# Attention in front of two layers of experts: 96-key spans, mask and log terms as contraction rows, and another order of TensorE's work

## The reference

```python
block, window = (32, 16)
k_sum = k.reshape(B, H, nb, block, D).max(axis=3)
v_sum = v.reshape(B, H, nb, block, D).mean(axis=3)
scores_l = scale * np.matmul(q, k.transpose(0, 1, 3, 2))
mask_l = np.abs(pos[:, None] - pos[None, :]) < window
scores_s = scale * np.einsum('bhsd,bhnd->bhsn', q, k_sum) + np.log(block)
scores_all = np.concatenate([np.where(mask_l, scores_l, -1e9), scores_s], axis=-1)
a = softmax(scores_all)           # the denominator has 1e-9 added
x = np.matmul(a, np.concatenate([v, v_sum], axis=2))
x = _moe_ref(x=x, **moe_kwargs)   # 3072 rows, 8 experts by argmax
return _moe2_ref(x=x, **moe2_kwargs)  # 3072 rows, 8 experts of equal capacity
```

## Time and profile before

| | us |
|---|---|
| median of 3 runs | 1345.78 |
| lowest and highest run | 1344.59 and 1348.11 |
| span of the profiled execution, first to last instruction | 1342.1 |
| the profiled execution's own time | not listed apart; the median is 3.7 above the span |
| start of the first row maximum (L1099) | 33.48 |
| start of the last `route` (L1124) | 358.34 |
| from there to the end | 983.8 |

### The profile page before, as it was taken

How to read it: one execution, slowest core, us unless ns; L and a number is a source line. 1 busy time by engine, 2 the same in 40 slices (tenths; PEclk the granted TensorE clock), 3 DMA queues, 4 the chain that set the end, 5 groups by cost and what they waited for, 6 DMA issues and landing times.

```text
span 1342.1 us, 24008 instructions
## 1 busy us (share of the span) xinstructions
PE 1034.3 (77%) x6788; PEld 843.7 (63%) x6789; DVE 684.5 (51%) x2047; ACT 476.9 (36%) x1393; POOL 193.3 (14%) x289
## 2 busy tenths in 40 slices
PE   2879798999637999999999522332325999999995
PEld 1658686777526888888888422222224888888884
DVE  5887676868464222222222377767773445445431
ACT  2758686979424122222212300000001344344330
POOL 4560000000010112121111100000001222222221
PEclk9989898989758999999999755555556999999998
DMA  6897896965365101111010110000002244443410
GB/s 119 171 130 84 76 110 70 104 72 77 32 206 194 48 32 44 34 39 39 32 47 32 37 54 0 0 0 0 0 0 87 102 173 164 164 165 127 150 36 23
DMA packets 128338, 103.25 MB, mean 77 GB/s; under 512 B 93329, under 2 KB 105761, under 8 KB 127521
## 3 DMA queue, kind: packets, MB, share of 16 engines
q1 hardware_dynamic: 119360, 71.39, 28.1%
q0 software_dynamic: 8928, 31.33, 7.3%
HBM read 82.98 MB, written 19.71 MB: 77 GB/s over the span
## 4 chain that ended last, share of the span: by engine, by line
PE 60%; issue 24%; DVE 7%; ACT 4%; DMA 2%; POOL 1%; SPq 0%; DVEq 0%; ACTq 0%; POOLq 0%
PE bank L714 38%; PE bank L639 3%; PE bank L738 3%; PE bank L662 2%; PE bank L663 2%; PE bank L721 2%; PE bank L674 1%; PE bank L761 1%; PE bank L625 1%; PE bank L648 1%; ACT probs L884 1%; PE bank L650 1%; PE bank L635 1%; PE bank L754 1%; DMA bias<-in_moe_modality_bias 1%
## 5 line engine op out<-in xcount | busy, mean ns | idle before, releaser
L714 PE MATMUL bank<-W,xh 128*128 (+1 forms) x784 | 255.1, 407 | 12.8 <-DVE gates L1237 10.0
L714 PE MATMUL bank<-W,hh 128*128 (+1 forms) x784 | 252.8, 404 | 10.4 <-DVE hl L1244 10.4
L714 PEld LDWEIGHTS bank<-W,xh 128*128 128x128 f32 x784 | 146.6, 192 | 45.7 <-issue 10.6
L714 PEld LDWEIGHTS bank<-W,hh 128*128 128x128 f32 x784 | 145.4, 190 | 42.7 <-issue 9.1
L714 PE MATMUL bank<-W,xl 128*128 (+1 forms) x392 | 156.8, 400 | 0.0
L714 PE MATMUL bank<-W,hl 128*128 (+1 forms) x392 | 156.1, 398 | 0.0
L934 ACT ACTIVATE xh<-bank 128x512 fp32r<-128x512 f32 x50 | 29.8, 595 | 269.5 <-PE bank L721 269.5
L805 PE MATMUL bank<-ge,cb 128*8 128x16 bf16 x1344 | 42.3, 172 | 106.8 <-DVE ge L1355 106.8
L1244 DVE TENSOR_TENSOR hl<-bank,hh 128x512 fp32r<-128x512 f32 x98 | 63.1, 685 | 96.1 <-ACT hh L934 91.6
L805 PEld LDWEIGHTS bank<-ge,cb 128*8 128x8 bf16 x1344 | 36.1, 83 | 112.0 <-DVE ge L1355 112.0
L559 POOL COPY gidx<-idx 128x1 int32 (+1 forms) x50 | 10.4, 209 | 644.0 <-DVEq L1187 530.6
(11 more groups left out here) (256 smaller groups left out, 1894.5 us busy)
## 6 DMA issues: line engine op xcount, KB each, us to landing
raw_w<-in_moe_w SPq DMA_DIRECT2D x20, 2048.0 KB, 10.1
qk_raw<-in_q SPq DMA_DIRECT2D x32, 192.0 KB, 7.9
qk_raw<-in_k SPq DMA_DIRECT2D x32, 192.0 KB, 8.6
vrow<-in_v POOLq DMA_DIRECT2D x6, 768.0 KB, 6.4
x_rows<-x SPq DMA_DIRECT2D x12, 384.0 KB, 10.4
va<-in_v SPq DMA_DIRECT2D x32, 100.0 KB
vb<-in_v SPq DMA_DIRECT2D x32, 100.0 KB
x_rows<-x SPq DMA_DIRECT2D x4, 387.0 KB, 10.0
```

The source lines that it names most:

```text
L714: last = mm(ps, lhs[a][:, c, :], rhs[b](c), start=c == 0 and t == 0, stop=c == n - 1 and t == 2)
```

## The change

- The host now lays q and k out transposed, with k cut into 12 overlapping spans of 96 keys for each head (64 queries and 16 keys on either side), and v cut into the same spans with a column of ones. `strips`, `strip_high` and `strip_low` are gone, with their buffers.
- q and k are plain float32. Partitions 0 to 63 hold the 64 dimensions; partitions 64 to 127 hold an identity on q's side and, on k's side, the mask and the log(32) term. So one float32 matmul of 64 queries against 120 columns (96 keys and 24 summaries, the new PW) gives a masked score. A unit has 4 of them; two write PSUM partitions 0 to 63, two write 64 to 127. The factor 1/8 moves into the exponential and into a new small DVE instruction on the maxima.
- The probabilities aren't normalised any more. They are transposed (2 transposes for 4) and used as weights, 64 columns at a time, against 65 columns of v: the result comes out as rows, with the sum of the row in the 65th. `normalise` reads both from PSUM and writes x; it now stands behind `values`. A transpose of x (`transpose_rows`) feeds the logits, in all units.
- `block_maxima` on DVE takes the maxima of a whole pair of heads in one reduction of 64 x 1536 elements and a copy of 64 x 576, once in 6 units, behind `normalise`.
- The block means of v: 1 chunk on DVE at the start, 7 on POOL; they no longer go through HBM but by 4 small transfers of each chunk, and POOL spreads them with one copy (24 x 1536 elements) for each pair of heads, 16 in all, each when the pair's buffer is free.
- SP: q and k of a pair arrive in 2 transfers (384 KB and 720 KB, both to 64 partitions), v in one (585 KB to 96 partitions). They are asked for when the scores, or values, of the pair two before are done.
- TensorE's order within a step: values n-3, transpose_rows n-4, logits n-5, transposes n-2, and scores of n last. LEAD is 6 for 5.

```diff
-WK = P + 2 * WINDOW
-HALF = WK // 2
-PA = HALF + NB
+
+
+
+
+QB = P // 2
+NQ = S // QB
+WK = QB + 2 * WINDOW
 PW = WK + NB
-TW = P + NB
-KW = 2 * WINDOW + QT * TW
-VARIANT = [0] + [1] * (QT - 2) + [2]
+VD = D + 1
...
-LEAD = 5
-
-TRANSPOSED = {0: 0, 1: 1, 3: 2}
-COPIED = {1: 0, 2: 1, 4: 2}
+LEAD = 6
...
+                sp.dma_start(qe[hp % 2][0:D, :, :], q[bass.ds(b, 1), hp, :, :, :].rearrange("o d h s -> (o d) h s")).then_inc(qk_loaded[hp % 2], 16)
+                sp.dma_start(kbt[hp % 2][0:D, :, :, :], k[bass.ds(b, 1), hp, :, :, :, :].rearrange("o d h j w -> (o d) h j w")
+                             ).then_inc(qk_loaded[hp % 2], 16)
+
+            def load_v(b, hp):
+                sp.dma_start(va[hp % 2][0:WK, :, :, :], v_win[bass.ds(b, 1), hp, :, :, :, :].rearrange("o p h j w -> (o p) h j w")
+                             ).then_inc(vw_loaded[hp % 2], 16)
...
             load_qk(0, 0)
+            sp.dma_start(vrow[0][:, :], v[0:96, :]).then_inc(vfirst_loaded, 16)
+            load_v(0, 0)
...
+                    def refill_qk(nb, nhp):
+                        sp.wait_ge(scores_done, UNITS * b + QT * (hp + 1))
+                        load_qk(nb, nhp)
...
+                        load_v(nb, nhp)
+
+                    for refill in (refill_qk, refill_v):
+                        if hp + 2 < HP:
+                            refill(b, hp + 2)
...
+            kr = [t[D:P, :, :, :].rearrange("p h j w -> p (h j) w") for t in kbt]
+            qr = [t[D:P, :, :].rearrange("p h (j u) -> p (h j) u", u=QB) for t in qe]
+            chain(g.memset(kr[0][:, :, WK:PW], math.log(BLOCK) / SCALE))
+            chain(g.memset(kr[0][:, :, 0:WK], 0.0))
+            chain(g.affine_select(out=kr[0][:, :, 0:WK], in_=kr[0][:, :, 0:WK], compare_op=ALU.is_ge, fill=MASKED, base=-1,
+                                  pattern=[[0, 2 * NQ], [1, WK]], channel_multiplier=-1))
+            chain(g.affine_select(out=kr[0][:, :, 0:WK], in_=kr[0][:, :, 0:WK], compare_op=ALU.is_ge, fill=MASKED,
+                                  base=2 * WINDOW - 1, pattern=[[0, 2 * NQ], [-1, WK]], channel_multiplier=1))
+            chain(g.memset(kbt[0][D:P, :, 0, 0:WINDOW], MASKED))
+            g.memset(kbt[0][D:P, :, NQ - 1, WK - WINDOW:WK], MASKED).then_inc(bias_rows, 1)
+            pool.wait_ge(bias_rows, 1)
+            chain(g.memset(qr[0], 0.0))
+            g.affine_select(out=qr[0], in_=qr[0], compare_op=ALU.not_equal, fill=1.0, base=0,
+                            pattern=[[0, 2 * NQ], [-1, QB]], channel_multiplier=1).then_inc(eye_rows, 1)
+            pool.wait_ge(eye_rows, 1)
...
+            def place_means(c):
+                for n in range(4):
+                    pool.dma_start(vst[c % 2][WK:PW, n // 2, n % 2, :], vmean[c % 2][NB * n:NB * n + NB, :]).then_inc(vmean_placed, 16)
...
+            def spread_means(c, half):
+                hp = 2 * c + half
+                if hp >= 2:
+                    pool.wait_ge(pv_done, QT * (hp - 1))
+                pool.wait_ge(vmean_placed, 64 * (c + 1))
+                ins = g.tensor_copy(va[hp % 2][WK:PW, :, :, 0:D], vst[c % 2][WK:PW, half, :, :].unsqueeze(2).to_broadcast([NB, 2, NQ, D]))
+                ins.then_inc(vsum_done, 1)
+
+            load_rows(1)
+            pool.wait_ge(vmean0_done, 1)
+            place_means(0)
+            load_rows(2)
+            spread_means(0, 0)
+            spread_means(0, 1)
+            for c in range(1, 8):
+                block_means(c)
+                if c >= 2:
+                    pool.wait_ge(vsum_done, 2 * (c - 1))
+                place_means(c)
                 if c + 2 < 8:
+                    load_rows(c + 2)
+                spread_means(c, 0)
+                spread_means(c, 1)
...
-                ps = bank[n % 2][:, 0:2 * PW].rearrange("p (h k) -> p h k", h=2)
-                mm(ps, identb[:, :], mask[:, VARIANT[i], :, :], start=True, stop=False)
-                mm(ps[:, :, HALF:PA], onesb[0:3, :], logb[:, :, :], start=False, stop=False)
-                cols = slice(TW * i, TW * i + PW)
-                for qp, kp in ((ql, kh), (qh, kl), (qh, kh)):
-                    last = mm(ps, qp[hp % 2][:, P * i:P * i + P], kp[hp % 2][:, :, cols], start=False, stop=qp is qh and kp is kh)
+                for h in range(2):
+                    for s_ in range(2):
+                        last = mm(bank[n % 2][QB * s_:QB * s_ + QB, PW * h:PW * h + PW], qe[hp % 2][:, h, P * i + QB * s_:P * i + QB * s_ + QB],
+                                  kbt[hp % 2][:, h, 2 * i + s_, :], start=True, stop=True)
                 last.then_inc(scores_done, 1)
...
             def transpose_probs(b, n):
-                pe.wait_ge(norm_done, UNITS * b + n + 1)
+                pe.wait_ge(exp_done, UNITS * b + n + 1)
                 if n >= 2:
-                    pe.wait_ge(pt_out[n % 2], UNITS // 2 * b + n // 2)
-                ps = bank[2 + n % 2]
+                    pe.wait_ge(pt_out, UNITS * b + n - 1)
                 for h in range(2):
-                    tr(ps[0:PA, P * h:P * h + P], probs[n % 3][:, h, 0:PA], ident[:, :])
-                for h in range(2):
-                    last = tr(ps[0:HALF, 256 + P * h:256 + P * h + P], probs[n % 3][:, h, PA:PW], ident[:, :])
+                    last = tr(bank[2 + n % 2][0:PW, P * h:P * h + P], probs[n % 3][:, h, :], ident[:, :])
                 last.then_inc(pt_done, 1)
...
+                for h in range(2):
+                    for s_ in range(2):
+                        last = mm(bank[4 + n % 2][QB * s_:QB * s_ + QB, VD * h:VD * h + VD], pt[n % 2][:, h, QB * s_:QB * s_ + QB],
+                                  va[hp % 2][:, h, 2 * i + s_, :], start=True, stop=True)
+                last.then_inc(pv_done, 1)
...
+            def transpose_rows(b, n):
 
                 hp, i = n // QT, n % QT
+                c = P * (hp % HP)
+                pe.wait_ge(x_done, UNITS * b + n + 1)
+                if n >= 2:
+                    pe.wait_ge(xt_out, UNITS * b + n - 1)
+                    if (n - 2) // QT % HP == HP - 1:
+                        pe.wait_ge(logits_out, QT * b + QT * ((n - 2) // UNITS) + (n - 2) % QT + 1)
+                tr(bank[6 + n % 2][:, 0:P], x[:, i, c:c + P], ident[:, :]).then_inc(xT_made, 1)
...
+            def first_logits(b, n):
+                hp, i = n // QT, n % QT
+                if hp % HP == HP - 1:
+                    pe.wait_ge(xt_out, UNITS * b + n + 1)
+                    m = QT * (hp // HP) + i
+                    if m >= 2:
+                        pe.wait_ge(logits_out, QT * b + m - 1)
                     for c in range(KC):
+                        last = mm(bank[6 + n % 2][:, P:P + E], xt[:, c, i, :], wg[:, c, :], start=c == 0, stop=c == KC - 1)
+                    last.then_inc(logits_made, 1)
...
-                t = TRANSPOSED.get(n % QT)
-                own(scores, n, n)
-                if t is not None:
-                    own(strips, n + QT, n // QT + 1, t)
-                if n >= 2:
-                    own(transpose_probs, n - 2, n - 2)
                 if n >= 3:
                     own(values, n - 3, n - 3)
                 if n >= 4:
-                    own(rows_of_x, n - 4, n - 4)
+                    own(transpose_rows, n - 4, n - 4)
+                if n >= 5:
+                    own(first_logits, n - 5, n - 5)
+                if n >= 2:
+                    own(transpose_probs, n - 2, n - 2)
+                own(scores, n, n)
...
+                if n >= 2:
+                    own(copy_probs, n - 2, n - 2)
                 if n >= 4:
                     own(copy_x, n - 4, n - 4)
-                if n % QT in COPIED:
-                    own(strip_high, n + QT, n // QT + 1, COPIED[n % QT])
-                if n >= 2:
-                    own(copy_probs, n - 2, n - 2)
                 own(exponentials, n, n)
+                if n >= 5:
+                    own(copy_logits, n - 5, n - 5)
...
+            def block_maxima(b, hp):
+
+                dve.wait_ge(qk_loaded[hp % 2], 64 * b + 32 * (hp // 2 + 1))
+                if hp >= 2:
+                    dve.wait_ge(ksum_done, HP * b + hp - 1)
+                own_keys = kbt[hp % 2][0:D, :, :, WINDOW:WINDOW + QB].rearrange("p h j (n t) -> p (h j) n t", t=BLOCK)
+                vec.tensor_reduce(ksum[hp % 2][:, :, :].rearrange("p h (j n) -> p (h j) n", n=2), own_keys, AXX, ALU.max).then_inc(bmax_done, 1)
+                dve.wait_ge(bmax_done, HP * b + hp + 1)
+                vec.tensor_copy(kbt[hp % 2][0:D, :, :, WK:PW], ksum[hp % 2][:, :, :].unsqueeze(2).to_broadcast([D, 2, NQ, NB])).then_inc(ksum_done, 1)
...
+                                  AXX, ALU.max, negate=True).then_inc(max_done, 1)
+                dve.wait_ge(max_done, UNITS * b + n + 1)
+                vec.tensor_scalar(nmax[n % 2][:, :], nmax[n % 2][:, :], SCALE, None, ALU.mult).then_inc(nmax_done, 1)
...
             def normalise(b, m):
+                hp, i = m // QT, m % QT
```

(29 more changed lines are left out.)

## The result

The changed kernel takes **1390.48 us** (median of four runs, 1387.95 to 1392.67) against 1345.18 before (four runs, 1342.14 to 1348.11): ratio 1.0336, 95% interval 1.0311 to 1.0361, slower. The forecast was 1358 with a range of 1318 to 1392. The side is right and the time is inside the range, but the loss is 45 us where 12 to 13 were forecast, so more than two thirds of it was not foreseen.

A forecast was written before the change was run, and what follows sets the result against it. TensorE bounds the kernel before; after the change, a serial circle of 2.69 us a unit. Terms sum to 337.7 against 324.9, 12.8 longer: 1342.1 + 12.8 + 3.7 = 1358.6, called 1358, range 1318 to 1392.

The forecast's parts named there:

- the circle: Each unit's scores wait through DVE's maxima and normalise and TensorE's transpose of x for the last unit's scores: 2.69 us.
- Block maxima: DVE's reduction and copy once a pair: 1.75 and 0.5 us, making the next scores wait 0.7, x 15 = 10.5.
- q and k late behind batch ends: At batch ends the next q and k land 4 us late behind the store of x: x 3 = 12, bounds 0 and 21.
- logits: Logits' weight loads on TensorE and their bank's copy lie inside the circle: 0.97 us x 19 units = 18.4.
- drain: From the last maximum to the route: 9 us, five steps of about 1.7, where it was 13.1.
- The clock term: TensorE at 1.2 GHz after gaps at POOL's sums and batch ends, some 6 more units than now: 7 us.
- The price of the scores: Four float32 score products of 120 columns on TensorE, 480 x 1.67 ns = 0.80 us, plus a tail of 0.17.
- POOL's share: POOL's sums slow DVE's scaling, 9.6 us, and its 16 spreading copies cost 9.6: together 19, bounds 8 and 35.
- Rival 1: Score products in the array's two halves run side by side: circle 2.39 us, time 1335, chance 0.29.
- Rival 3: TensorE's clock stays low in the attention: 1476 us if all units at 1.2 GHz, 1397 if a third; chance 0.13.
- Rival 2: No circle because normalise is ready early; TensorE bounds at about 2.1 us a unit: 1313 us, chance 0.08.
- rival 4: q and k come late to every pair's block maxima: 2.8 us x 15 = 42 more, 1400 us, chance 0.07.

The follow-up runs named there:

- e1: Changed kernel with DVE's normalise of unit n-3 put ahead of the maxima of unit n: 1343.15 us, ratio 0.9987.
- e11: Changed kernel with 150 bf16 products of 128 columns on TensorE ahead of the attention: 1390.26 us, ratio 1.0330.
- e2: Changed kernel with TensorE's order as in the kernel before (newest scores first), DVE's list kept: 1301.41 us, ratio about 0.967.
- e3: Changed kernel with six unused bf16 products of 128 columns on TensorE after values in every unit: 1359.06 us, ratio 1.0115.
- e10: Changed kernel with 128 queries as weights in each score product, writing 128 partitions; no longer computes the attention: 1392.14 us, ratio 1.0346.
- e8: Changed kernel with score products ordered lower, lower, upper, upper half of the PSUM partitions instead of alternating: 1393.49 us, ratio 1.0352.
- e12: e7 with DVE's maxima put back ahead of normalise, as in the changed kernel: 1374.94 us, ratio 1.0217.
- e6: e1 with block maxima two units later and the last pair's x stored after the requests for the next q and k: 1294.73 us, ratio 0.9621.
- e7: e6 with ACT's copy of the logits ahead of the exponentials: 1271.49 us, ratio 0.9463.
- e9: e7 with six unused bf16 products of 128 columns on TensorE in each unit: 1258.88 us, ratio 0.9353.
- e13: e9 with ten unused bf16 products in each unit in place of six: 1266.75 us, ratio 0.9426.

## Why the prediction was off

The prediction had the mechanism of the loss, the circle, and its side right; the size failed, above all by the clock.

**Right.** The circle: its place, its members, their order, and that every unit pays it. Its DVE part was costed at 1.28 and is 1.29. Block maxima: 1.75 and 0.5 costed, 1736 and 502 ns measured; they lengthen a plain step by 0.86 (0.7 forecast). q and k late behind batch ends: 12 forecast, 8.8 us of waits measured (one of the four, of 0.55 us, is not at a batch end), k landing in 7.3. That a pair's k is in time in general: yes, at the pace of the circle; at a faster pace (e1) not. DVE as the engine that TensorE waits for at `transpose_rows`: yes.

**The steps that failed**, against the sum of 337.7, where the trace has 368.7 (357.24 + 14.9 - 3.4):

| term | forecast | measured | off by |
|---|---|---|---|
| 95 circles | 95 x 2.69 = 255.6 | 95 x 3.20 = 304.0 | +48.4 |
| logits | 19 x 0.97 = 18.4 | 19 units, 33.1 over 3.20 each | +14.7 |
| block maxima, POOL, batch ends, late k, clock | 54.2 | 20.2 | -34.0 |
| drain | 9 | 14.9 | +5.9 |
| start | 0.5 | -3.4 | -3.9 |

They add up to +31.1, 0.1 by rounding; the third line holds the two first steps too, which are shorter than 3.20. Behind the route come 4.6 us that the text said would not be there.

1. *The clock term, "some 6 more such units than now: 7".* This is the step that failed. It had all but a few units at 2.4 GHz; all of them ran at 1.2. It was weighed against one window, 2.96 of 4 busy at 1.00, in a kernel whose work was of another kind. In the changed kernel 28.7 of 40 are busy at 1.2 GHz (e11), and in e2 36.4 of 40 at 0.70: one row of another kernel could not carry this term. The prediction's own sign, "the granted clock at 1.00 in the middle of pairs", was met on record and still did not show 2.4 GHz. The price: 3.20 - 2.46 = 0.74 a unit, 95 x 0.74 = 70.3, and for the logits the products behind eight weight loads of 128 columns at 1.72 (the row at 207.86), where the loads had 0.97 at full clock: 0.75 x 19 = 14.3, about their whole error. Both prices are worked out from single steps; no run shows the whole attention at full clock with the circle. Raising the clock by filler alone gave 31 in e3, where it was at 0.78 from 60 to 300 us.
2. *The price of the scores, "480 x 1.67 = 0.80".* Taken from a float32 product with 128 columns of weights. With 64 columns a pass of 120 moved columns goes at some one cycle a column and not two: eight passes take 0.63 at full clock (e3) and sixteen 1.04 (e11), so 0.051 for one, and with 128 columns of weights eight take 1.05 (e10). Scores and their tail are thus 0.63 where 0.97 was costed, and 0.10 comes back between the transposes and the scores (see the rivals). By e3 the circle at full clock is 2.46 and not 2.69, 95 x 0.23 = 22 less. This hid part of the first error: 70.3 - 21.9 = 48.4. That the forecast missed by 32 us and not by more is in part this luck.
3. *Side terms.* POOL's share was put at 19, for its sums and its spreading copies together, and came to 92 x (238 - 170) ns = 6.3 on the scaling. The spreading copies took 1.47 for 1.8. Block maxima in the units with logits cost only 0.2 (steps of 5.12 for 4.92), since ACT's copy holds the unit anyway; the sum had 0.7 for each of 15.
4. *The drain.* Five steps at 1.7 were costed at full clock; it took 14.9 at 1.2 GHz, and the logits of the last units stand in it; how the 5.9 divide was not separated.

**The rivals.** Rival 1 had the right size for the wrong reason: circle 2.39 forecast, 2.46 at full clock in e3, but not by halves side by side, as far as e8 shows. The Trainium skill ("TensorEngine Tiling (Array Packing)", Key Properties) says that tiles can load and multiply in parallel. No run here shows two of these products at once, and for this order and this type e8 speaks against it. The same section says that a change of tiling mode drains TensorE. That rule fits: ahead of the 64-column loads TensorE's loader idles 0.34 us at 1.2 GHz (92 times, 31.1 us) and 0.17 at 2.4, and in e10, where transposes and scores both have 128 columns, the idle time there is gone (it stands ahead of the values' loads instead, 9.7 us in all). It costs the circle 0.34 - 0.24 = 0.10 at full clock, where I had 0.17. Rival 3, the low clock in all units, is what happened; it was priced at 1476, because it doubled scores that were already priced too dear, and given 0.13. Rival 2, no circle, was wrong, and rival 4 is what the kernel becomes once the circle is cut (e1).

**Left open.** Why the clock stays low is not shown: the filler shows that more products bring it up, not which property of them. The prediction also said that nothing would move behind the route by more than 3 us, and 4.6 did. The timeline has a place for 3.4 of them. The copy of the row numbers for the second gather of tokens, POOL's, starts 35.55 us behind the route after the change and 35.53 before it. It then takes 4.52 us where it took 1.11, and TensorE waits 4.2 us for the gather in place of 0.9. After, with what DVE does beside it, and then before:

```profile
437.62 4.62 DVE L1130 TENSOR_TENSOR W<-raw_w,W 128x1024 fp32r<-128x1024 f32 x4
437.77 4.52 POOL L513 COPY gidx<-idx 128x1 int32<-128x1 int32 x1 [12.09 <-DVE gates L1136]
```

```profile
393.72 4.62 DVE L1231 TENSOR_TENSOR W<-raw_w,W 128x1024 fp32r<-128x1024 f32 x4
393.87 1.11 POOL L559 COPY gidx<-idx 128x1 int32<-128x1 int32 x1 [12.08 <-DVE gates L1237]
```

After the change POOL's copy ends 0.05 us behind the last of DVE's four products of the weights, before it 0.04 us behind the first (one takes 1.22). e8 and e12, the other two kernels with 988 us from the route to the end (988.1 and 988.3), have 4.51 for this copy; e11 (984.8) and e1, e2, e3, e6, e7, e9, e10 and e13 (983.1 to 984.9) have 1.11. Why the copy comes in behind the first or the fourth product is open. It may differ from one execution to the next: the changed kernel's four spans are 1390.6 and 1390.9, 1386.6 and 1386.1. Only the first of them has a trace, so that isn't shown.

## What to carry to other kernels

Write each engine's list beside the others' and look for a path from the newest unit's first stage back to itself one unit later: its length is a floor for the unit, whatever the engines' busy shares say, and putting oldest work first on an engine that waits for an engine doing newest work first closes such a path. Behind a circle the next limits are hidden (here the transfer of k, the copy of the logits, the clock), so undo them together: e1 alone gave 47 us, e1, e6 and e7 together 119. And read the clock off the length of a known instruction, not off the clock's record or the engine's busy share alone.

## What the runs showed of the hardware

- A granted clock of 1.00 was on record for about 370 us in which every product had the length that it has at 0.50 (e11).
- A float32 product's pass with 64 weight columns takes about half of one with 128: eight passes of 120 columns 0.63 (e3) and 1.05 us (e10) at 2.4 GHz, with the same latency in both. At 1.2 GHz eight loads of 64 columns with their 65-column products took 0.65 (values), eight loads of 128 columns with 8-column products 1.72 (logits).
- Six small bf16 products in a unit, none of whose results is used, made the kernel faster: 31 us in e3 and 12.6 in e9. Ten gave 4.7 over e7 (e13).
- DVE's scaling of 128 x 2 elements took 238 ns in the mean and 170 where it met no work of POOL's; the longest took 1.42 us.
- A copy of 128 elements on POOL took 1.11 or 4.5 us beside DVE's products of 128 x 1024 elements, and ended 0.04 to 0.05 us behind the first or the fourth of them.
- The Trainium skill ("SBUF — State Buffer", Door 1) gives 196 GB/s for 1 MiB to partitions 0 to 63; the 720 KB of k landed in 7.3 us from the issue, 0.1 MB a us with its latency and q's transfer beside it, which doesn't contradict it.
